# Gate and token number carried in each x row, expert outputs stored in expert order, final rows scattered

## The chip, the cores and the metric

The kernel runs on one core of a Trainium2 chip. The metric is device time of one execution, in microseconds (us), as the median of three runs. All arithmetic is float32 or float32r; each large product is made as three float32r matmuls of high and low parts.

## The reference

```python
# attention over 32 packed tokens, two softmax stages, 8 batches x 8 heads x 576 tokens x 64
p_packed = sm_attn(p, k, v)
out = sm_attn(q, p_packed, p_packed)
x = out.transpose(0, 2, 1, 3).reshape(4608, 512)
# one expert of eight for each token
logits = x @ w_gate                                   # 4608 x 8
expert_idx = argmax(logits); gate_w = softmax(logits)[expert_idx]
for e in range(8):                                    # 512 -> 1024 -> 512
    out[mask_e] = gate_w[mask_e] * (maximum(x[mask_e] @ w1[e], 0) @ w2[e])
# dense block, 512 -> 2048 -> 512
r = maximum(x @ w_in, 0); y = (s * r * r + b) @ w_out
```

## The kernel before

The program is written engine by engine, with semaphores by hand. It has three stages one behind another.

**Attention** (0 to about 185 us). Sixteen units of four heads, software-pipelined in iterations over PE (TensorE), ACT (ScalarE), DVE (VectorE) and POOL (GpSimd). A batch is two units. After each batch POOL sums its logits, DVE's `experts(b)` (L1011) picks the expert of each token by a chain of small instructions, PE ranks the tokens (`ranks`), DVE's `positions(b)` (L1030) turns ranks into row numbers, and POOL's `scatter` (L410) writes the x rows, 96 at a time and 2048 bytes each, to `x_by_expert` in DRAM: eight regions of 4736 rows. 48 such scatters run in all.

**Expert slots** (about 205 to 716 us). A slot is 128 rows of one expert; here there are 40. Behind the last tokens DVE works out tables (first slot of each expert, DRAM row of each slot), and the rows behind the last token of each region are filled with zeros: four DMAs from SP's queue (L345) and four from ACT's (L867), at addresses loaded from the table. ACT waits for all scatters and all zero rows before it loads slot 0 (`load`, L873 to L876). In the loop PE runs `slot_up(s)`, `slot_in(s + 1)`, `slot_down(s - 1)`, `slot_turn(s)`; ACT runs `relu(s)`, `x_hi(s + 1)`, `load(s + 2)`, `y_out_(s - 1)`, `h_hi(s)`; DVE makes the low parts (`x_lo`, `h_lo`). `y_out_` copies y out of PSUM and stores it at the slot's own row of `y_by_slot`. Eight chunks of the next expert's weights are split into high and low parts by POOL (`split`, L390) when an expert's buffer is released. In parallel, gate values and slot rows of all tokens are computed once and go through DRAM (`gate_dram`, `pos_dram`) so that they can be read back in token order.

**Dense** (about 725 us to the end). Nine groups of four tiles of 128 tokens. POOL gathers the y rows of a tile by token (`gather_y`, L452), ACT multiplies them by the gate (`scale`, L947), PE transposes them (`tile_in`, L723), ACT and DVE make high and low parts, then PE runs 16 blocks per group of `dense_up` and `dense_down`, 12 matmuls each. Block n needs a relu on ACT, a square on DVE (L1217), a high part on ACT (L962) and a low part on DVE (L1219). Gathers of later groups lie inside the group before. The output of a group is in token order: each partition holds four consecutive tokens, and SP writes it with one DMA of 1 MB (L367). The last weights, `w_out`, can be split only when the last slot's product is done (`release(E + 1)`).

The handover to the dense stage on ACT ends with these lines, and POOL waits for `y_all` before its first gather:

```python
y_out_(before3 + 2)
act.wait_ge(y_out, (before3 + 4) * 16)
act.sem_inc(y_all, 1)
```

## Time and profile before

| | |
|---|---|
| median of 3 runs | 1571.49 us (1571.23 to 1572.86) |
| profiled execution | 1566.7 us, of which the span of instructions is 1564.9 us |
| PE busy | 1471.0 us, 94% of the span |
| DVE, ACT, POOL busy | 471.2, 473.2, 411.2 us |
| DMA | 124.57 MB, mean 80 GB/s |
| the chain that ended last | PE 91% of it |

How to read it: PE is the engine that sets the time, so what counts is where PE is idle or runs at its lower clock. A window row gives the busy time of each engine in a stretch with its number of instructions, the granted clock as a share of 2.4 GHz, the busy share of the 16 DMA engines and the GB/s that they moved.

### The profile page before, as it was taken

The page shows a single profiled execution, that of the slowest core. Times are in us where ns is not written, and L with a number is a line of the kernel's source. Part 1 is how long each engine was busy: PE and PEld are TensorE (multiplying, and loading weights), DVE is VectorE, ACT ScalarE, POOL GpSimd, SP SyncE. Part 2 cuts the span into 40 slices and gives each one's busy share as a digit, 9 for nine tenths or more (in the row PEclk, how much of TensorE's full clock was granted, in tenths as well). Part 3 has the DMA queues.
Part 4 walks back from the last instruction along what each step waited for, and adds up shares of the span by engine and source line. Part 5 has one row for each costly group of instructions (what it writes and reads, how often), then busy time and mean ns, then how long its engine had stood idle before and what let it go on. Part 6 is the DMA issues. An engine that isn't in the chain of part 4 may idle for free.

```text
span 1564.9 us, 24350 instructions
## 1 busy us (share of the span) xinstructions
PE 1471.0 (94%) x8664; PEld 1177.8 (75%) x8665; DVE 471.2 (30%) x776; ACT 473.2 (30%) x809; POOL 411.2 (26%) x269
## 2 busy tenths in 40 slices
PE   7888369999999999995999999999999999999998
PEld 5556258888888888884788888888888888888886
DVE  3766631111111111111523232332323233232322
ACT  5655122222222222222222232322223232222222
POOL 0344568448266547006500000000000000000000
PEclk9998679999999999997999999999999999999999
DMA  8887464234233333113101010010101001000000
GB/s 260 252 263 226 136 207 161 85 107 135 75 132 107 112 123 121 67 35 108 55 8 40 14 40 7 13 40 8 39 13 40 7 13 40 8 32 0 27 1 27
DMA packets 51906, 124.57 MB, mean 80 GB/s; under 512 B 8224, under 2 KB 14368, under 8 KB 50720
## 3 DMA queue, kind: packets, MB, share of 16 engines
q1 hardware_dynamic: 31904, 83.13, 16.4%
q10 hardware_dynamic: 14016, 22.10, 4.3%
q0 software_dynamic: 5952, 18.88, 3.8%
q8 instruction: 22, 0.36, 0.1%
q14 instruction: 12, 0.10, 0.0%
HBM read 90.76 MB, written 33.33 MB: 79 GB/s over the span
## 4 chain that ended last, share of the span: by engine, by line
PE 91%; issue 3%; ACT 2%; DVE 1%; DMA 1%; POOL 0%; SPq 0%; another core or an unknown queue 0%; ACTq 0%; DVEq 0%; POOLq 0%
PE psum L660 18%; PE psum L662 18%; PE psum L661 18%; PE psum L740 9%; PE psum L742 9%; PE psum L741 9%; PE psum L493 2%; PE psum L704 2%; PE psum L728 1%; PE psum L669 1%; PE psum L554 1%; PE psum L533 1%; PE psum L608 1%; PE psum L563 0%; ACT a1T L805 0%
## 5 line engine op out<-in xcount | busy, mean ns | idle before, releaser
L1217 DVE SCALAR_TENSOR_TENSOR s_r_r<-r_relu,s_col 128x512 f32<-128x512 f32 x144 | 112.9, 784 | 453.2 <-ACT r_relu L959 453.2
L660 PE MATMUL psum<-weights_split,gT_hi 128*128 128x512 f32 x576 | 230.6, 400 | 1.9 <-DVE gT_lo L1219 1.9
L740 PE MATMUL psum<-yT_hi,weights_split 128*128 128x512 f32 x576 | 228.4, 396 | 1.4 <-issue 1.4
L741 PE MATMUL psum<-yT_lo,weights_split 128*128 128x512 f32 x576 | 228.5, 397 | 0.0
L742 PE MATMUL psum<-yT_hi,weights_split 128*128 128x512 f32 x576 | 228.4, 396 | 0.0
L662 PE MATMUL psum<-weights_split,gT_lo 128*128 128x512 f32 x576 | 228.0, 396 | 0.0
L661 PE MATMUL psum<-weights_split,gT_hi 128*128 128x512 f32 x576 | 227.6, 395 | 0.0
L959 ACT ACTIVATE r_relu<-psum 128x512 f32<-128x512 f32 x144 | 86.0, 597 | 465.5 <-PE psum L742 465.5
L395 POOL TENSOR_TENSOR weights_split<-weights_raw,one 128x1024 fp32r<-128x1024 f32 x70 | 134.7, 1925 | 252.8 <-PE psum L662 236.5
L457 POOL DMA_INDIRECT y_gathered<-y_by_slot,tpos x36 | 34.4, 957 | 580.1 <-PE psum L728 578.2
L397 POOL TENSOR_TENSOR weights_split<-weights_raw,weights_split 128x1024 fp32r<-128x1024 f32 x70 | 169.2, 2417 | 5.5
L1219 DVE SCALAR_TENSOR_TENSOR gT_lo<-s_r_r,b_col,gT_hi 128x512 fp32r<-128x512 f32 x144 | 112.9, 784 | 114.1 <-ACT gT_hi L962 114.1
L962 ACT ACTIVATE gT_hi<-s_r_r,b_col 128x512 fp32r<-128x512 f32 x144 | 104.3, 724 | 123.4 <-DVE s_r_r L1217 123.4
L660 PE MATMUL psum<-weights_split,xT_hi 128*128 x320 | 130.7, 408 | 2.9 <-DVE xT_lo L1188 2.9
L660 PE MATMUL psum<-weights_split,hT_hi 128*128 x320 | 129.8, 406 | 2.5 <-DVE hT_lo L1194 2.5
L740 PEld LDWEIGHTS psum<-yT_hi,weights_split 128*128 128x128 f32 x576 | 108.5, 188 | 28.0 <-issue 1.8
L660 PEld LDWEIGHTS psum<-weights_split,gT_hi 128*128 128x128 f32 x576 | 108.2, 188 | 27.5 <-issue 2.1
L741 PEld LDWEIGHTS psum<-yT_lo,weights_split 128*128 128x128 f32 x576 | 108.5, 188 | 26.9
L742 PEld LDWEIGHTS psum<-yT_hi,weights_split 128*128 128x128 f32 x576 | 108.7, 189 | 26.3
L662 PEld LDWEIGHTS psum<-weights_split,gT_lo 128*128 128x128 f32 x576 | 108.1, 188 | 26.1
L661 PE MATMUL psum<-weights_split,xT_hi 128*128 x320 | 127.1, 397 | 0.0
L662 PE MATMUL psum<-weights_split,xT_lo 128*128 x320 | 126.9, 397 | 0.0
(143 smaller groups left out, 1786.3 us busy)
## 6 DMA issues: line engine op xcount, KB each, us to landing
weights_raw<-in_moe_w_dram SPq DMA_DIRECT2D x64, 512.0 KB, 3.5
x_slot<-x_by_expert ACTq DMA_DIRECT2D x40, 256.0 KB, 2.7
y_by_slot<-y_slot ACTq DMA_DIRECT2D x40, 256.0 KB, 2.0
k_sb<-in_k_dram SPq DMA_DIRECT2D x16, 576.0 KB
q_sb<-in_q_dram SPq DMA_DIRECT2D x16, 576.0 KB, 7.2
v_sb<-in_v_dram SPq DMA_DIRECT2D x48, 192.0 KB
out_dram<-out_sb SPq DMA_DIRECT2D x9, 1024.0 KB, 3.9
weights_raw<-in_moe_w_in_dram SPq DMA_DIRECT2D x8, 512.0 KB, 3.7
```

Of the source, the lines that this page charges most:

```text
L395: nc.gpsimd.tensor_tensor(hi, raw[c_ % 2][:], one[:].to_broadcast([P, CH]), ALU.mult).then_inc(hi_done, 1)
L397: nc.gpsimd.tensor_tensor(lo, raw[c_ % 2][:], hi, ALU.subtract).then_inc(conv, 1)
L660: nc.tensor.matmul(dst, lhs[0][:, col:col + P], rhs[0], start=first_, stop=False)
L661: nc.tensor.matmul(dst, lhs[0][:, col:col + P], rhs[1], start=False, stop=False)
L662: return nc.tensor.matmul(dst, lhs[1][:, col:col + P], rhs[0], start=False, stop=last_)
L740: nc.tensor.matmul(ps[:, HFB + f % 2, :], w[0], yT[0][:, k_, :], start=(k_ == 0), stop=False)
L741: nc.tensor.matmul(ps[:, HFB + f % 2, :], w[0], yT[1][:, k_, :], start=False, stop=False)
L742: last = nc.tensor.matmul(ps[:, HFB + f % 2, :], w[1], yT[0][:, k_, :], start=False, stop=(k_ == KD - 1))
L959: nc.scalar.activation(rel[:], ps[:, HFB + par, :], ACT.Relu).then_inc(rel_done, 1)
L962: nc.scalar.activation(gT[par][0][:], sq[par][:], ACT.Identity, bias=b_col[:]).then_inc(ghi_done, 1)
L1217: nc.vector.scalar_tensor_tensor(sq[par][:], rel[:], s_col[:], rel[:], ALU.mult, ALU.mult).then_inc(sq_done, 1)
L1219: nc.vector.scalar_tensor_tensor(gT[par][1][:], sq[par][:], b_col[:], gT[par][0][:], ALU.add, ALU.subtract).then_inc(glo_done, 1)
```

## The change

The last two columns of a longer x row (514 floats, 2056 bytes) hold the gate and the token's output row number. The gate is computed batch by batch in the attention stage. A y row (513 floats, 2052 bytes) is scaled when it leaves PSUM and carries the row number. The y rows are stored without gaps in expert order: a slot that would reach beyond its expert's last token starts earlier, so that no padding rows are read (as long as an expert has 128 tokens or more). The dense stage reads contiguous tiles with plain DMAs, and its result rows are scattered to the output by POOL. Zero rows are written once, at the head of each region, before the attention loop. The first four tiles are loaded, transposed and split while the last slots are still in work.

```diff
-    rows_dram = nc.dram_tensor("x_by_expert", [E * REG, DM], F32).ap()
-    ys_dram = nc.dram_tensor("y_by_slot", [SLOTS * P, DM], F32).ap()
-    pos_dram, gate_dram = ...
+    rows_dram = nc.dram_tensor("x_by_expert", [E * REG, XW], F32).ap()   # XW = DM + 2
+    ys_dram = nc.dram_tensor("y_sorted", [N + P, YW], F32).ap()          # YW = DM + 1
@@ SP, after the attention loads
-            sp.wait_ge(rt, RT_PAD)
-            for e in range(E // 2):
-                row = sp.value_load(pad_row[0:1, e:e + 1], ...)
-                sp.dma_start(rows_dram[bass.ds(row, P), :], zeros[:]).then_inc(zeroed, 16)
-            sp.dma_start(ys_dram[N:SLOTS * P, :]..., zeros[:]...).then_inc(tail_zero, 16)
@@ SP, dense
+            for c_ in range(2):
+                chunk(c_, (E + 1) * NCH + c_, w_out_chunk(c_))
+            sp.wait_ge(y_out, before3 * 16 + 16)
+            for i in range(GT):
+                load_y(1, i)
+            for c_ in range(2, NCH):
+                chunk(c_, (E + 1) * NCH + c_, w_out_chunk(c_))
+            for g in range(2, GROUPS):
+                for i in range(GT):
+                    load_y(g, i)        # waits for ty_full of the tile before
-            with sp.Fori(0, GROUPS) as g:
-                sp.dma_start(out_v[:, bass.ds(g, 1), :], osb[:]...).then_inc(out_done, 16)
@@ POOL scatter
+                if j0 == 0:
+                    nc.gpsimd.tensor_copy(x_rows[:, b % XBUFS, :, DM + 1], ids[:, b, :]).then_inc(ids_done, 1)
@@ POOL, end
-            (gather_y(0), split 1, gather_y(1), splits 2 to 7, gather_y(2 to 8))
+            for c_ in range(NCH):
+                split(c_, (E + 1) * NCH + c_, WBUF)
+            for g in range(GROUPS):
+                for i in range(GT):
+                    pool.wait_ge(o_dve if i % 2 else o_act, 2 * g + 3 + i // 2)
+                    nc.gpsimd.indirect_dma_start(out, IndirectOffsetOnAxis(ap=out_row[:, t:t + 1], axis=0), osb[:, i, :], None)
+                pool.wait_ge(out_done, 16 * GT * (g + 1))
+                pool.sem_inc(osb_free, 1)
@@ PE, end of the slots
             slot_up(before3 + 2)
+            tile_in(0, 0)
+            tile_in(0, 1)
             slot_down(before3 + 1)
+            tile_in(0, 2)
+            tile_in(0, 3)
             slot_turn(before3 + 2)
             slot_down(before3 + 2)
-            for i in range(GT):
-                tile_in(0, i)
@@ ACT
+            act.dma_start(rows_dram.rearrange("(e r) c -> r e c", e=E)[0:P],
+                          zeros[:].unsqueeze(1).to_broadcast([P, E, XW])).then_inc(zeroed, 16)
+                if it >= 5 and it % 2 == 1:
+                    exp_logits((it - 5) // 2)
-            def y_out_(s):
+            def y_out_(s, age):
+                nc.scalar.copy(ysb[:, DM:], gid[age][:, 1:2])
-                nc.scalar.copy(ysb[:], ps[:, YB, :]).then_inc(y_done, 1)
+                nc.scalar.activation(ysb[:, 0:DM], ps[:, YB, :], ACT.Copy, scale=gid[age][:, 0:1]).then_inc(y_done, 1)
                 act.wait_ge(y_done, s + 2)
+                row = act.value_load(y_at[0:1, bass.ds(s, 1)], min_val=0, max_val=N)
+            def keep_columns(s, n):     # n copies of 128x2 between three buffers, then one out of x_slot
@@ DVE
@@ experts(b)
+                nc.vector.tensor_tensor(shifted[:], lgb, mx[:]..., ALU.subtract).then_inc(exp_in, 1)
+            def gates(b):               # at the head of positions(b)
+                nc.vector.reduce_sum(psum_e[:], powers[:], AX.X)
+                nc.vector.tensor_scalar_add(psum_e[:], psum_e[:], EPS)
+                nc.vector.reciprocal(x_rows[:, b % XBUFS, :, DM], psum_e[:])
```

Three places in the order of instructions (a wait on a semaphore stands in brackets; x3 is three in a row).

ACT between attention and slots, before. The names: `x_slot` is the tile of slot 0, `el` and `dl` belong to the gates of all tokens.

```order
L867 DMA x_by_expert<-zeros 128x512
L901 TENSOR_LOAD slots_minus [waits tables]
L875 TENSOR_LOAD slot_row [waits x_sent3,x_sent2,zeroed,x_sent1,x_sent0]
L876 DMA x_slot<-x_by_expert 128x512
L829 CAST weights_split<-weights_raw 128x1024 [waits raw_in0]
L829 CAST weights_split<-weights_raw 128x1024 [waits raw_in1]
L910 ACTIVATE el<-dl 96x384 [waits rt]
L880 CAST xT_hi<-psum 128x512 [waits tx_full]
```

The same place of the changed kernel.

```order
L832 ACTIVATE logits_exp<-logits_shifted 96x48 [waits exp_in] x2
L912 TENSOR_LOAD slots_minus [waits tables]
L876 TENSOR_LOAD slot_row [waits x_sent2,x_sent3,x_sent1,x_sent0]
L877 DMA x_slot<-x_by_expert 128x514
L828 CAST weights_split<-weights_raw 128x1024 [waits raw_in0]
L828 CAST weights_split<-weights_raw 128x1024 [waits raw_in1]
L881 CAST xT_hi<-psum 128x512 [waits tx_full]
L908 COPY gate_and_token<-x_slot 128x2
```

The zero DMAs and the wait on `zeroed` are gone from here; two small exponentials stand in their place.

PE from the last slot's `slot_up` to the dense stage, before: `xT` rows are `slot_up`, `hT` rows `slot_down`, `h_relu` rows `slot_turn`.

```order
L704 MATMUL psum<-ident,h_relu 128x128 [waits hlo_done,relu_done]
L704 MATMUL psum<-ident,h_relu 128x128 x3
L660 ISA [waits y_done,hlo_done,conv]
L660 MATMUL psum<-weights_split,hT_hi 128x512
...
L728 MATMUL psum<-ident,y_gathered 128x128 [waits yg_scaled]
L728 MATMUL psum<-ident,y_gathered 128x128 x3
L728 MATMUL psum<-ident,y_gathered 128x128 [waits ylo_done,yg_scaled]
L740 MATMUL psum<-yT_hi,weights_split 128x512 [waits rel_done,ylo_done,conv]
```

The same of the changed kernel.

```order
L719 MATMUL psum<-ident,y_tile 128x128 [waits row_read]
L719 MATMUL psum<-ident,y_tile 128x128 x3
...
L657 ISA [waits y_done,hlo_done]
L657 MATMUL psum<-weights_split,hT_hi 128x512
...
L719 MATMUL psum<-ident,y_tile 128x128 [waits ylo_done,row_read]
...
L701 MATMUL psum<-ident,h_relu 128x128 [waits hlo_done,relu_done]
...
L657 ISA [waits y_done,hlo_done,conv]
...
L731 MATMUL psum<-yT_hi,weights_split 128x512 [waits rel_done,ylo_done,conv]
```

The sixteen transposes of group 0 moved ahead of the last slot's `slot_down`, eight before and eight after that of the slot before it.

ACT over the same stretch in the changed kernel, from the load of the four tiles on; before, the copies to `y_slot` were followed directly by the DMA and by `hT_hi`.

```order
L939 DMA y_tile<-y_sorted 128x513 x4
L891 CAST hT_hi<-psum 128x512 [waits th_full] x2
L886 ACTIVATE h_relu<-psum 128x512 [waits h_full]
L946 CAST out_row_of_y<-y_tile 128x1 [waits yg_in0]
...
L950 CAST yT_hi<-psum 128x4x128 [waits ty_full] x2
L897 COPY y_slot<-gate_and_token 128x1 [waits y_out]
L898 ACTIVATE y_slot<-psum,gate_and_token 128x512
L900 TENSOR_LOAD slot_y_row
L901 DMA y_sorted<-y_slot 128x513
L950 CAST yT_hi<-psum 128x4x128 [waits ty_full] x2
L891 CAST hT_hi<-psum 128x512 [waits th_full] x2
```

Ahead of the last `hT_hi` there now stand the load of a row number and two more `yT_hi`.

## Rows read from the trace of the kernel before

**Rows 1.** Busy time by stretch, core 0.
```profile
160.00:200.00 40.00, 11.47 (x240) 9.11 (x237) 21.83 (x71) 3.90 (x7) 21.57 (x25) 0.58 0.50 156
200.00:240.00 40.00, 29.77 (x133) 23.98 (x134) 14.83 (x17) 10.75 (x18) 30.21 (x15) 0.82 0.58 185
500.00:600.00 100.00, 100.00 (x482) 81.95 (x481) 15.84 (x24) 26.70 (x48) 56.04 (x27) 1.00 0.34 110
700.00:720.00 20.00, 13.26 (x61) 10.30 (x59) 1.29 (x2) 2.84 (x5) 4.07 (x2) 0.98 0.07 27
```

**Rows 2.** The chain that ended last, slots to dense: start, length, what.
```profile
707.80 0.59 ACT hT_hi L890
...
709.92 0.49 PE psum L660
...
715.53 0.25 PE psum L662
...
744.59 0.48 PE psum L660
```

**Rows 3.** Timeline around the second last slots: start, length, engine, line.
```profile
694.59 0.59 ACT L896 COPY y_slot<-psum 128x512 f32<-128x512 f32 x1 [5.04 <-PE psum L662]
696.35 1.29 DVE L1194 TENSOR_TENSOR hT_lo<-psum,hT_hi 128x512 fp32r<-128x512 f32 x2 [6.08 <-ACT hT_hi L890]
700.97 0.60 ACT L885 ACTIVATE h_relu<-psum 128x512 f32<-128x512 f32 x1 [2.20 <-PE psum L662]
706.37 1.03 PE L704 MATMUL psum<-ident,h_relu 128*128 128x128 f32 x8
743.75 2.34 POOL L395 TENSOR_TENSOR weights_split<-weights_raw,one 128x1024 fp32r<-128x1024 f32 x1
744.27 2.38 DVE L1217 SCALAR_TENSOR_TENSOR s_r_r<-r_relu,s_col 128x512 f32<-128x512 f32 x1
```

**Rows 4.** Small operations by line, or a line's own answer: count, durations.
```profile
L821 ACT COPY pkx<-psum 128x8 f32<-128x8 f32 x16 | 2.5, 158 | 0.5 <-PE psum L544 0.5
L950 ACT ACTIVATE y_gathered<-y_gathered,tgate 128x512 f32<-128x512 f32 x36 | 25.6, 711 | 7.9 <-DMA y_gathered<-y_by_slot,tpos 7.9
L875 ACTq TENSOR_LOAD <-slot_row x40: 274/277/994, 199.9 to 676.5; - x40
```

**Rows 5.** Attention to slots: the last scatter (timeline), then the chain.
```profile
192.93 0.92 POOL L414 DMA_INDIRECT x_by_expert<-x_rows,row_of_token_sb  x1 [0.30 <-issue]
...
195.84 4.01 DMA x_by_expert<-zeros
...
201.33 5.97 DMA x_slot<-x_by_expert
...
210.06 0.79 PE psum L660
```

**Rows 6.** DMAs issue to landing: of x_slot, of y_gathered, and two issues by line.
```profile
DMA to landing us min/median/max: 2.4/2.7/6.0
DMA to landing us min/median/max: 3.1/3.3/4.0
y_by_slot<-y_slot ACTq DMA_DIRECT2D x40, 256.0 KB, 2.0
out_dram<-out_sb SPq DMA_DIRECT2D x9, 1024.0 KB, 3.9
```

**Rows 7.** Attention: chain of one odd iteration, and two stretches of its start.
```profile
91.56 0.22 DVE eq L1019
...
25.00:30.00 5.00, 4.02 (x82) 3.22 (x80) 2.18 (x5) 2.90 (x5) 0.00 (x0) 0.87 0.26 91
10.00:15.00 5.00, 3.44 (x40) 2.53 (x38) 1.18 (x2) 2.87 (x5) 0.00 (x0) 1.00 1.07 320
```

**Rows 8.** The end: last copy of a result tile (timeline), and POOL's gathers by line.
```profile
1559.75 0.69 DVE L1226 COPY out_sb<-psum 128x512 f32<-128x512 f32 x1 [0.64 <-PE psum L662]
...
L457 POOL DMA_INDIRECT y_gathered<-y_by_slot,tpos x36 | 34.4, 957 | 580.1 <-PE psum L728 578.2 <-issue 1.7
```

271 lines of the change are left out of this document (132 added, 139 removed).

## The prediction

> **What bounds the kernel now.** I read the windows by stage first. In the middle of the slots PE is busy 100.00 of 100 us at granted clock 1.00, so nothing is won there by work taken off other engines. PE is idle in two places: between attention and slots (11.47 us busy of 40, then 29.77 of 40) and between slots and dense (13.26 busy of 20 in the first half of that gap) [rows 1]. The dense stage behind it is as full as the slots: the product chain there is PE's alone. Then I read the chain that ended last across both gaps, and the timelines for what each engine does in them.
>
> In the second gap the turn of the last slot begins at 706.37 [rows 3]; PE starts the last y product at 709.92, ends it at 715.78, and starts the first dense down product at 744.59 [rows 2]. In between stand the store of y, a weight split on POOL, the gather, and four rounds of scale, transpose and copy one behind another, none overlapped. In the first gap the last scatter starts at 192.93, the last zero DMA at 195.84 and lands 4.01 us later, slot 0's load starts at 201.33, takes 5.97 us, and PE's first slot product starts at 210.06 [rows 5].
>
> All sums are made against the profiled execution: 1566.7 us, its span 1564.9 us. The median of the three runs is 1571.49, 4.8 us more; I add my difference to that median.
>
> **Slots to dense, the main term.** New timetable, on the old trace's clock. PE ends `slot_up` of the last slot as before; its second relu runs 700.97 to 701.57 [rows 3]. The first tile's transposes wait for that relu and a cast of 128x1, priced as the 128x8 copy at 0.158 [rows 4], so they start at 701.8, 1.1 after PE was free. Eight transposes cost 1.03 like the eight of the turn [rows 3]. That puts `slot_down` of the slot before last 2.1 later: its end moves from 706.4 to 708.5. Two more tiles (1.03) and the turn (1.03) follow, then PE waits for `h_lo`. On ACT: 0.1 to see the product, 0.16 for the row-number column, 0.71 for the scaled copy (the scale of a y tile has the same shape, 0.711 [rows 4]), 0.17 for its semaphore, a row load of 0.28 [rows 4] with about 0.4 of register work, 0.35 for the DMA, two `yT_hi` of 0.59 like the y copy [rows 3]: `hT_hi` starts 3.35 after the product. Before, it took 2.12 from there to PE's start (707.80 to 709.92 [rows 2]); I add 0.2 because DVE has `y_lo` to finish. Last y product: starts 714.2, takes 5.86, ends 720.1. The two dense up blocks take 5.6 (24 matmuls, like the y product without its start) and end at 725.7.
>
> The first down block cannot start then: its relu, square, high and low part need 3.0 us after the first up block, and POOL is splitting `w_out` from 720.2 on. In the trace a DVE instruction with both inputs in SBUF that started at 744.27, during a POOL split that ran from 743.75 to 746.09, ended at 746.65, 2.38 instead of 0.75 [rows 3]: it waited for the POOL instruction to end. With splits of 1.9 and 2.35 in turn the square and the low part each lose about a microsecond: down starts at 727.3. Against 744.59 that is **17.3 us gained**. Bounds: 19.8 with no POOL wait and one microsecond less on ACT; 12.7 with both waits at 2.38, half a microsecond more on ACT, and PE's clock down after the idle stretch.
>
> That last point is open. PE is now idle for some 3.6 us in one piece, where before a 2.5 us piece at 707.4 left the clock at 0.98 over its stretch [rows 1] and the long gap lowered it. A fall would cost 12 matmuls 0.2 us each, 2.4 in all. I leave it out of the sum and keep it in the range.
>
> **Attention to slots.** Zero rows and the wait on them are gone from here. The last scatter starts 0.4 later (POOL copies ids, one small instruction and its semaphore), 193.3. Its landing is not shown. The gather of the same queue and nearly the same size lands in 3.3 (3.1 to 4.0), a plain store of y in 2.0 [rows 6]; I take the gather's 3.3, since the queue is the same. With 0.7 for the row load, slot 0's load starts at 197.4. Its 5.97 was in company of zero stores and weights; the median is 2.7 [rows 6], and now the stores are gone and weight chunk 9 came earlier: 200.1. From landing to PE's first product 2.7 as before: 202.8 against 210.06, **7.2 us gained**. Bounds: 8.5 with landing in 2.0; 3.2 if scatter and load take 4.0 and 6.0.
>
> The table step on DVE grows by five or so instructions of 0.2 on one partition; it ended before the last scatter was issued and has until that lands, so it costs nothing. Without that cover it would cost 1 us.
>
> **Attention loop.** `experts(b)` stands on the chain, one small DVE instruction after another at 0.22 to 0.24 [rows 7]. One more is added, for seven batches inside the loop: **1.7 us lost**. The three of `gates(b)` (0.6 together) go between an x copy and the turn of the packs, behind which DVE waited for PE in the iteration that I followed (90 to 105 us), so they are hidden; unhidden they would cost 0.6 x 7 = 4.2. The exponential on ACT falls into a wait for PE.
>
> The zero rows are written at 12 us: 1024 rows of 2056 bytes, 2.1 MB. DMA moves 320 GB/s with a share of 1.07 there, but at 25 to 30 us the share is 0.26 [rows 7], and k, q, v are loaded an iteration ahead. I take **0.5 us lost**, including ACT's time to issue it; 0 if it is all hidden, 2.1 MB / 0.29 = 7.2 if not at all.
>
> **Slot loop.** Zero. ACT gets per slot three copies of 0.16, the column, 0.12 more in the scaled copy and a row load: about 1.8 us. The one path that matters is y product, y copy, `h_hi`, `h_lo`: its low parts ended at 697.64, and PE wants them at about 701.3, after `slot_up` and `slot_in` [rows 3]. The path grows by 0.95 and had 3.7 to spare.
>
> **Dense loop and end.** Gathers leave POOL, tile loads leave from SP, ACT saves 0.55 per tile, POOL scatters. None is on PE's chain, and osb is free 80 us before it is wanted. Zero. If the scatter of a group were held up, PE would wait only from 80 us on. At the very end SP's 1 MB store landed 3.9 after its issue [rows 6], 0.2 after the last copy ended at 1560.44 [rows 8]. Now POOL issues four scatters, 0.957 each [rows 8] with 0.3 between; tiles come every 0.8, so the fourth starts at about 1562.15 and lands 2.6 to 3.3 later, 1564.75 to 1565.45 against 1564.55. I take **0.6 lost**, -0.4 to 1.6.
>
> **Sum.** -17.3 - 7.2 + 1.7 + 0.5 + 0.6 = -21.7 us. The span goes to 1543.2, the profiled execution to 1545.0, the median to 1549.8.
>
> **Two rules weighed.** Above, the zero store was hidden by the gap in DMA traffic at 25 us. The Trainium skill (DMA: Bandwidth & Descriptors, Issuing engines are not separate DMA queues) says that DMAs from any engine share the same 16 DMA engines and interleave, so ACT's queue buys nothing but issue time. By that rule alone the sum would be -21.7 + 6.7 = -15.0. Whether loads are late for it no row before can show; that is rival A.
>
> The x rows grow by 0.4% in bytes. The same page (How a descriptor splits into AXI transactions) says that a descriptor that does not start on a 256-byte boundary is cut into more transactions; nearly every 2056-byte row starts off one. By it the estimate is some 10% more DMA work for the scatters, 0.06 MB per batch or 0.2 us, 1.8 us if attention were bound by DMA. No run so far shows it.
>
> **Rivals.**
> A. *Attention is held by DMA.* DMA engines stood at a share of 1.07 just when the zero store would be issued [rows 7]. If loads come late, the zero store costs up to 7.2 and longer rows 1 or 2 more. For it: the share. Against it: in the waits of the loop PE is released by ACT and DVE, hardly ever by a load. Time: 1549.8 + 4 to 8 = 1554 to 1558. Chance 0.2.
> B. *The handover is worse than my timetable*: clock falls (2.4), POOL blocks DVE for two or three blocks more (1.5 each), scatter lands late (2). For it: the 2.38 row. Time 1553 to 1557. Chance 0.13.
> C. *Slower.* ACT's longer round in the slot loop reaches PE. It decides once the path y product to `h_lo` grows by more than 3.7 us per slot; then each microsecond beyond costs 37. A row load once took 0.99 instead of 0.277 [rows 4], which would bring the growth to 1.7, still 2 short. One microsecond beyond gives 1549.8 + 37 = 1587. Chance 0.03.
> D. *The gap is moved, not closed.* The tiles' loads or the new waits (SP's on y stores, PE's on `row_read`) hold PE before the last slot's products, and the first gap is set by scatters that land no sooner: gains of 3 and 3 instead of 24. About 1568. Chance 0.04.
> The forecast itself: 0.6, with its own range 1546.5 to 1553.5.
>
> **Numbers.** Predicted 1549.8. 80% range: from 1545.5 (bounds 19.8 and 8.5, no losses but 1.7) to 1558 (rivals A and B inside). 0.2%, about 3.1 us, is what a measurement of this kernel can tell. Faster 0.94, same 0.02, slower 0.04.
>
> **What the changed kernel's profile would show.** Slots to dense: from the end of the second last y product to the first down product about 18.8 us instead of 38; a PE idle piece of 3 to 4 us before the last y product, its releaser `hT_lo`; clock 1.00 through it. Attention to slots: `x_slot` load about 3.5 to 4 us after the last scatter, landing in 2.7. Attention: iterations with `experts` 0.2 longer, the last scatter about 2.5 later than 192.93. Slots: windows still 100.00 of 100. End: last scatter issued at about 1.7 after the last copy. I am wrong if the attention stage is more than 5 us longer, if PE has idle time between slots 5 and 35, or if the first down product waits more than 3 us for `gT_lo`.

## The result and the profile after

The changed kernel takes 1560.22 us (median of 4 runs, 1558.07 to 1561.81) against 1571.41 for the kernel before on the same chip: ratio 0.9928, interval 0.9915 to 0.994. It is 11.2 us faster, where 21.7 was forecast, and lies above the range. The profiled execution took 1560.72 us, its span 1559.0, against 1566.7 and 1564.9: 5.9 us less by the pair of profiles. The profile of before had caught a quick execution, 4.8 us under its median. One of ten later executions of the kernel before (run before_again) took 2110.83 us at a granted clock of 0.648 and is left out of that run's ratio.

I cut both traces at five marks: the start of the last scatter, the start of the first slot product, the start of the last relu of the slots, the start of the first dense down product, the end of the last result copy. In us:

| stretch | before | after | difference | forecast | difference of means |
|---|---|---|---|---|---|
| attention, to the last scatter | 192.93 | 204.13 | +11.2 | +2.6 | +9.5 |
| to the first slot product | 17.13 | 9.61 | -7.5 | -7.6 | -8.2 |
| slots, to the last relu | 490.91 | 492.69 | +1.8 | 0 | +0.9 |
| to the first dense down product | 43.62 | 29.12 | -14.5 | -17.3 | -15.5 |
| dense, to the last result copy | 815.85 | 811.51 | -4.3 | 0 | -4.6 |
| end | 4.46 | 11.94 | +7.5 | +0.6 | +7.5 |
| sum | | | -5.8 | -21.7 | -10.4 |

The last column takes four profiles of before or of near variants of it (before, before_again, before_zero, before_aligned) and five of the changed kernel (after, after_again, end_nowait, end_plain, handover; handover only up to the last relu, and of the end only after and after_again). Two of the four have an edit in a stage of the table: without before_zero the attention difference is +9.1; without before_aligned the one to the first dense down product is -14.9 and the dense one -5.0. The means add up to -10.4, next to the measured -11.2. Two profiles of one kernel differ by 1 to 3 us in the attention stage alone, so a single pair would have left 5 us unexplained here.

Busy time by stretch in the changed kernel (as in rows 1):

```profile
160.00:200.00 40.00, 20.48 (x405) 15.95 (x403) 29.18 (x99) 9.74 (x20) 21.21 (x26) 0.63 0.31 95
200.00:240.00 40.00, 26.12 (x112) 20.88 (x113) 9.18 (x19) 9.70 (x21) 29.15 (x16) 0.76 0.48 149
500.00:600.00 100.00, 100.00 (x481) 81.63 (x480) 15.85 (x24) 31.86 (x81) 55.71 (x28) 1.00 0.36 115
700.00:720.00 20.00, 15.09 (x80) 12.07 (x77) 4.83 (x8) 7.37 (x18) 0.00 (x0) 1.00 0.43 132
720.00:740.00 20.00, 17.37 (x67) 13.78 (x68) 7.21 (x5) 3.39 (x7) 11.68 (x6) 0.91 0.18 60
```

In the slots PE is still busy 100.00 of 100, with ACT at 31.86 us instead of 26.70 [rows 1]: ACT's longer round doesn't reach PE. The second gap, between slots and dense, has shrunk to one idle piece. The clock stays at 1.00 up to 720 and is 0.91 in the stretch behind.

The chain across the first gap, from the attention stage to the slots (start, length, what; as in rows 5):

```profile
204.13 3.40 DMA x_by_expert<-x_rows,row_of_token_sb
...
208.34 2.65 DMA x_slot<-x_by_expert
...
213.74 0.79 PE psum L657
```

Landing 3.40 for the scatter (3.3 taken from the gather), 2.65 for the load (2.7 taken): this term was read rightly.

The chain across the second gap (as in rows 2), then the last copy and the last scatter in the timeline (as in rows 8):

```profile
715.07 0.87 PE psum L719 x8
715.94 0.87 PE psum L701 x8
716.81 3.78 issue
720.59 0.49 PE psum L657
...
722.15 0.43 PE psum L658
...
731.43 1.58 DVE s_r_r L1224
...
733.80 1.52 DVE gT_lo L1226
...
735.55 0.47 PE psum L657
```

```profile
1546.37 0.69 DVE L1233 COPY out_sb<-psum 128x512 f32<-128x512 f32 x1 [0.64 <-PE psum L659]
...
1548.98 0.96 POOL L465 DMA_INDIRECT out_dram<-out_sb,out_row_of_y  x1 [0.30 <-issue]
```

The last copy ends at 1547.06. The last scatter starts 1.92 later, about as forecast (1.7). But the span ends only at 1559.0. The windows of the changed kernel (columns as in rows 1) say that nothing is left to do for most of that:

```profile
1550.00:1552.00 2.00, 0.00 (x0) 0.00 (x0) 0.00 (x0) 0.00 (x0) 0.00 (x0) 0.66 0.35 131
1552.00:1558.00 6.00, 0.00 (x0) 0.00 (x0) 0.00 (x0) 0.00 (x0) 0.00 (x0) 0.50 0.00 0
```

No engine works and no DMA moves from 1552 on. Two things thus had to be explained above all: the 7.5 us at the end, and 6.9 us more than forecast in attention.

### The profile page after: what moved, and what is told of

Its sections match the earlier page's. It is cut to its first block, busy times and chain, and to the rows that moved or that the text cites. A ratio compares the mean times of both kernels' runs of the same rounds, so it can differ in the third digit from the quotient of the medians.

```text
span 1559.0 us, 24694 instructions
## 1 busy us (share of the span) xinstructions
PE 1468.7 (94%) x8664; PEld 1181.3 (76%) x8665; DVE 474.2 (30%) x808; ACT 480.7 (31%) x973; POOL 416.0 (27%) x278
## 4 chain that ended last, share of the span: by engine, by line
PE 90%; DVE 3%; issue 2%; DMA 1%; ACT 1%; POOL 1%; another core or an unknown queue 0%; SPq 0%; ACTq 0%; DVEq 0%; POOLq 0%
PE psum L657 18%; PE psum L659 18%; PE psum L658 18%; PE psum L733 8%; PE psum L732 8%; PE psum L731 8%; PE psum L701 2%; PE psum L490 2%; PE psum L666 1%; PE psum L719 1%; PE psum L551 1%; PE psum L530 1%; PE psum L592 1%; DMA q_sb<-in_q_dram 1%; PE psum L605 1%
## 5 line engine op out<-in xcount | busy, mean ns | idle before, releaser
L1224 DVE SCALAR_TENSOR_TENSOR s_r_r<-r_relu,s_col 128x512 f32<-128x512 f32 x144 | 116.2, 807 | 449.5 <-ACT r_relu L955 449.5
L465 POOL DMA_INDIRECT out_dram<-out_sb,out_row_of_y x36 | 35.6, 990 | 746.9 <-ACT out_sb L965 738.6
L657 PE MATMUL psum<-weights_split,hT_hi 128*128 x320 | 130.8, 409 | 4.7 <-issue 4.7
L1206 DVE TENSOR_TENSOR hT_lo<-psum,hT_hi 128x512 fp32r<-128x512 f32 x80 | 51.6, 686 | 265.4 <-ACT hT_hi L891 265.4
L658 PE MATMUL psum<-weights_split,hT_hi 128*128 x320 | 127.1, 397 | 0.0
```

The costliest lines, as they stand in the source:

```text
L657: nc.tensor.matmul(dst, lhs[0][:, col:col + P], rhs[0], start=first_, stop=False)
L658: nc.tensor.matmul(dst, lhs[0][:, col:col + P], rhs[1], start=False, stop=False)
L1224: nc.vector.scalar_tensor_tensor(sq[par][:], rel[:], s_col[:], rel[:], ALU.mult, ALU.mult).then_inc(sq_done, 1)
```

## Experiments

Each run has its median and its ratio to runs of the kernel before on the same chip, with the 95% interval of the ratio. In one of the five series (pad160, before_moved, gates_late, two_edits) the attention stage ran nearly throughout at the upper clock, and all kernels were some 20 us shorter, the kernel before at a median of 1549.35; those four are compared with each other and by their ratios.

### How far one profile may be trusted

**before_again** is the kernel before, unchanged, profiled once more.

> The kernel before, once more, as a yardstick. Its profiled execution took 1566.7 us and its timed runs 1571.2 to 1572.9. If the profiled one was simply a fast one, the runs here spread between 1566 and 1573 and their granted clock with them (0.966 for the profiled one); if the profile differs by a fixed mechanism, all timed runs stay at 1571 to 1573 and the clock or one stage shows why. In the profile I expect the last scatter at 193 and the last result copy to end 4.5 us before the span does.

1571.53 us, ratio 0.9991 (0.9977 to 1.0006); the last scatter starts at 195.93 instead of 192.93, the handover to the dense stage takes 45.65 instead of 43.62. **after_again** is the changed kernel, unchanged.

> The changed kernel once more, on the same chip as the run below, since two profiles of one kernel differ by up to 3 us in the attention stage, and a whole series can lie 20 us from another with the clock. Theory: ratio to the kernel before 0.9928 as before, within 0.0015; 11.9 us at the end, 29.1 at the handover, 811.5 to 812 in the dense stage, whatever the clock does in the attention stage. If the attention stage runs at its upper clock nearly throughout, as it did in the last series, the gate costs the loop more, some 1.1 us a batch, and the ratio is 0.994 to 0.995.

1558.32 us, 0.9913 (0.9898 to 0.9929); last scatter at 203.44, end 11.95. The ratio of the change stands; the stages move by a few microseconds between executions, the end doesn't.

### The end

**end_nowait** takes away POOL's wait for its last four scatters; SP waits for them anyway.

```diff
-                pool.wait_ge(out_done, 16 * GT * (g + 1))
-                pool.sem_inc(osb_free, 1)
+                if g < GROUPS - 1:
+                    pool.wait_ge(out_done, 16 * GT * (g + 1))
+                    pool.sem_inc(osb_free, 1)
```

> The changed kernel with POOL's last wait for its own scatters left out (SP alone waits for them before the end; nobody needs osb any more). In the trace of the changed kernel the last scattered bytes moved at 1551.9, but the span ends at 1559.0, and SP waited 7.0 us for another engine's end. Theory 1 (POOL has something to do at its end that takes about 7 us, and it can start only when its wait is over): the end now starts 3 us earlier and the time is 1557. Rival 1 (what takes 7 us begins when the last scatter has landed, whoever waits): 1560, no change. Rival 2 (the 7 us are the wait of POOL itself for its semaphore): the span ends 1 us after the last bytes, 1553.5.

**end_plain** stores the last group by one plain DMA of SP instead, without a scatter; POOL's last scatter lies 80 us earlier.

```diff
+            sp.wait_ge(o_act, 2 * GROUPS + 2)
+            sp.wait_ge(o_dve, 2 * GROUPS + 2)
+            sp.dma_start(out[(GROUPS - 1) * GT * P:GROUPS * GT * P, :]..., osb[:]).then_inc(sb_in, 16)
...
-            for g in range(GROUPS):
+            for g in range(GROUPS - 1):
```

> The changed kernel with the last group written by one plain DMA of 1 MB from SP instead of POOL's four scatters (its 512 rows land in the wrong places of the output). POOL's last scatter is then that of the group before, 80 us from the end. Theory (POOL is late because its program ends only some 7 us after its last scatter has run): from the end of the last copy to the end of the span it takes 4.5 us as in the kernel before, instead of 11.9, and the time is 1560.2 - 7.5 = 1552.7. Rival (the 7 us come from something else in the new ending, such as SP's wait on 36 scatters): 11 us and 1559.

end_nowait: 1557.63 us, 0.9911 (0.9888 to 0.9934), from last copy to span end 10.07. end_plain: 1552.89 us, 0.9875 (0.9825 to 0.9924), 4.87 from last copy to end, about as in the kernel before (4.46). SP's queue waits (releaser, total us, count, longest), first of the changed kernel:

```profile
SPq L62 <- PEq L62: 7.0, 1, 7.0
```

then of end_nowait:

```profile
SPq L62 <- PEq L62: 5.2, 1, 5.2
```

then of end_plain:

```profile
SPq L372 <- DMA out_dram<-out_sb: 3.9, 1, 3.9
...
SPq L62 <- PEq L62: 0.2, 1, 0.2
```

L62 is the end of the program, where the engines wait for each other. In the kernel before this wait is 0.2 as well. The row names PE's queue, but PE's last matmul had started at 1545.94. What the wait is for shows in the instructions of line 62 on POOL's queue (duration in ns, start in us), of the changed kernel:

```profile
L62 POOLq DRAIN  x1: 6932/6932/6932, 1551.8 to 1551.8; - x1
```

of end_nowait:

```profile
L62 POOLq DRAIN  x1: 9769/9769/9769, 1545.1 to 1545.1; - x1
```

of end_plain:

```profile
L62 POOLq DRAIN  x1: 6606/6606/6606, 1466.4 to 1466.4; - x1
```

and of the kernel before, with POOL's last gather (timeline):

```profile
L62 POOLq DRAIN  x1: 8112/8112/8112, 1367.2 to 1367.2; - x1
...
1367.41 0.94 POOL L457 DMA_INDIRECT y_gathered<-y_by_slot,tpos  x1 [21.88 <-PE psum L728]
```

In end_nowait POOL's last scatter begins here (timeline):

```profile
1546.95 0.96 POOL L465 DMA_INDIRECT out_dram<-out_sb,out_row_of_y  x1 [0.30 <-issue]
```

In line 62 this DRAIN stands ahead of the last two semaphore instructions of POOL's queue. In the changed kernel it starts when the wait for the landing is over, at 1551.8, lasts 6.9 us, and the span ends 0.2 later. In end_nowait it is in the queue early and ends 6.9 us after the last scatter (1547.91 to 1554.9), again 0.2 before the span's end; the last scatter had landed by 1549.7, so the 6.9 us don't run from the landing. Dropping the wait let them start 2 us earlier and saved 1.9. In the kernel before the same DRAIN ends 6.9 us after the last gather (1368.36 to 1375.3), 190 us before the end, and in end_plain 79 us before it; there nobody waits for it. So POOL needs some 6.9 us behind its last gather or scatter before the program can end. What it does in them the trace doesn't show, and since POOL's last work is a gather or a scatter in every kernel here, no run shows whether other work would leave the same.

### Attention: the gates

**no_gates** leaves out the shift, the exponential and the three instructions of `gates`.

```diff
+                        nc.gpsimd.memset(x_rows[:, b % XBUFS, :, DM], 1.0)     # b < XBUFS
-                    exp_logits((it - 5) // 2)
-                nc.vector.tensor_tensor(shifted[:], lgb, mx[:]..., ALU.subtract).then_inc(exp_in, 1)
-                gates(b)
```

> The changed kernel without the gate's arithmetic in the attention stage: no shifted logits, no exponential, no sum, epsilon and reciprocal (the gate column is a constant 1 set four times by POOL, so the expert outputs are not scaled). Theory 1 (all four DVE instructions of a batch stand on the loop's chain, 0.8 us a batch, and 1.4 in the drain): last scatter at 204.1 - 6.5 = 197.6, time 1553.5. Rival, my prediction's term (only the one in experts is on the chain): 1.7 less, last scatter at 202.4, time 1558.5. Rival 2 (the loop is held by loads that come late): nothing changes, 204.

1555.24 us, 0.9887 (0.9864 to 0.991), where the changed kernel has 0.9928 and 0.9913: 4 to 6.5 us less by the ratios. The last scatter starts at 200.83. I split the stage by loads of v: to that of unit 7, from there to unit 15 (four batches), and to the last scatter.

| | before (mean of 4) | changed (mean of 5) | no_gates | three_edits |
|---|---|---|---|---|
| to v of unit 7 | 64.5 | 68.3 | 70.3 | 68.6 |
| units 7 to 15 | 81.7 | 84.1 | 81.6 | 81.1 |
| to the last scatter | 47.6 | 50.8 | 49.0 | 49.2 |

The first row scatters between 66.9 and 69.6 in the five profiles of the changed kernel, and the middle row between 80.1 and 84.2 in the four of before, so a single profile says little here; no_gates and three_edits (described below, with two of the gate's instructions fewer) agree in the middle row. Read by these means, the gates are the whole of the middle row's 2.4 and more than half of the last row's 3.2: some 4.4 us, against 1.7 forecast, with a few us of uncertainty.

The changed kernel's own chain (start, length, what) holds the three instructions of `gates` four times, here first:

```profile
124.99 0.12 DVE sum_of_exp L1044
...
125.13 0.18 DVE sum_of_exp L1046
...
125.33 0.19 DVE x_rows L1049
```

The others begin at 145.59, 167.28 and 184.79, and the shift of the logits is on the chain five times at 0.20: 3 us in all. In the iteration around 104 us the three are not on it, and DVE waits 1.14 us for PE behind them, as in the one that the prediction had followed. So they are hidden in some batches and not in others.

**gates_late** moves `gates` behind the turn of the packs, where DVE had waited for PE in the iteration that I had followed. **two_edits** is the changed kernel with end_nowait's and handover's edits, its gates unchanged.

```diff
@@ gates_late
-                gates(b)                      # at the head of positions(b)
...
+                if it >= 5 and it % 2 == 1 and it < UNITS + 2:
+                    gates((it - 5) // 2)      # behind turn_packs(it - 2)
```

> The changed kernel with the sum, the epsilon and the reciprocal of the gate moved behind DVE's transpose of the packs, where DVE waits 1.1 us for PE, instead of ahead of it; the last batch's stay ahead of its positions. POOL's scatters wait for them. Without the gate's arithmetic the loop took 20.4 us a batch instead of 21.0, and 49.0 instead of 50.9 from the last v load to the last scatter. Theory 1 (the three cost because they delay the transpose and what waits for it): a batch 20.6, last scatter 201.5, time 1558. Rival (they cost wherever they stand, or the shifted logits in experts are what costs): a batch 21.0, last scatter 203.3, time 1560.

> The changed kernel with the two edits that helped alone and leave the tiles where they are: the last h ahead of tiles 2 and 3 at the handover, and no last wait on POOL. 29.1 becomes 28.2 and 11.9 becomes 10.1: time 1557.4, ratio to the kernel before 0.991, and 0.989 if the better medians of the two runs alone (0.9895 and 0.9911) mean more than their profiles.

gates_late 1540.04 us, 0.9943 (0.9924 to 0.9963), last scatter at 185.34; two_edits 1535.05 us, 0.9923 (0.9894 to 0.9952), 180.22. Behind the turn the gates do no better. two_edits has two savings at other places that gates_late lacks, some 3 us or 0.0019, and the four middle batches take 68.7 us in it against 70.9 in gates_late. The chain of two_edits shows what the gates hold up:

```profile
94.52 0.76 DVE nm L1066
95.28 0.86 DVE x_rows L1113
96.14 0.12 DVE sum_of_exp L1045
...
96.28 0.18 DVE sum_of_exp L1047
...
96.48 0.19 DVE x_rows L1050
...
97.10 0.79 DVE a2T L1091
...
99.13 1.25 PE psum L593 x48
```

The three instructions stand between an x copy and `a2T`, which PE's 48 matmuls wait for. In this iteration, at the upper clock, DVE has no wait to spare.

**gates_pool** has POOL make shift, sum and reciprocal, for all batches but the last, with tiles of 224 bytes more:

```diff
+                nc.gpsimd.tensor_tensor(half[:], powers[:, :, 0:4], powers[:, :, 4:8], ALU.add).then_inc(pool_sum, 1)
+                ...                                       # quarter, whole, + EPS, pow(-1)
-                gates(b)
+                if b == B - 1:
+                    gates(b)
```

> The changed kernel with the gate's arithmetic of the first seven batches on POOL (one subtraction, three additions, epsilon, a power of -1; the exponential stays on ACT; the last batch stays on DVE), and the row numbers written into the x rows one step ahead, out of the way of the scatters. Theory 1 (what the four DVE instructions and POOL's copy cost is their place on DVE's and POOL's chain; without the arithmetic at all the last scatter came at 200.8 instead of 203.3 on average): last scatter at 200 to 201, time 1557. Rival (POOL's five instructions hold DVE's, as its splits do, or delay the scatters): last scatter at 203 or later, time 1560 or more.

1565.28 us, 0.9958 (0.9944 to 0.9973): last scatter at 204.94, no sooner than with the work on DVE. **best** is gates_pool with the edits of end_nowait and handover.

> The three edits together on the changed kernel: the gates on POOL, the last h ahead of tiles 2 and 3 at the handover, and no last wait on POOL. The handover edit alone gave 28.2 us from the last relu to the first down product instead of 29.1, the edit of the end 10.1 us from the last copy to the end of the span instead of 11.9. If they add up to what the gates give: 1560.2 - 3 - 1 - 1.9 = 1554.3, ratio to the kernel before 0.989. Rival (the gates on POOL give nothing): 1557.3, ratio 0.991.

1560.24 us, 0.9937 (0.9922 to 0.9953), last scatter at 204.58. My expectation that POOL had room fell. Why POOL's scatters are no sooner was not taken apart. Both kernels also lost 4.5 to 5.6 us in the dense stage (817.15 and 816.02), of which below.

### Attention: the zero rows and the longer rows

**zero_spread** writes the zeros by eight DMAs from SP's queue between the loads of units 2 to 5; **zero_spread2** does the same and lets POOL wait for them only before its first scatter.

```diff
+                if u <= 5:
+                    for e in (2 * u - 4, 2 * u - 3):
+                        sp.dma_start(rows_dram[e * REG:e * REG + P, :], zeros[:]).then_inc(zeroed, 16)
-            act.dma_start(rows_dram.rearrange("(e r) c -> r e c", e=E)[0:P], ...)
```

> The changed kernel with the same zero rows written by eight DMAs of 0.26 MB from SP, two behind the loads of each of the units 2 to 5, instead of one DMA of 2.1 MB from ACT at 12 us. Theory 1 (the single big store delayed the q load of unit 2, which took 11.8 us, and with it the loop by about 3 us): PE no longer waits for q at 33 us, the last scatter starts at 201 instead of 204.1 and the time is 1557, 3 less. Rival (the bytes themselves cost, wherever they are written, since the DMA engines are the limit of the loop): last scatter at 203.5 to 204.5, time 1560.

> As the kernel that spread the zero rows over eight DMAs behind the loads of units 2 to 5, but POOL waits for them only before its first scatter and no longer before it sums the logits of batch 0. In the first version that wait held POOL until 55.9 us (18.3 us idle) and the fifth load mark came 3 us later than in the changed kernel. Theory 1 (the big store delayed the loads and with them the loop by about 3 us; spread out it costs 1): v load of unit 6 issued at 54 to 55 us instead of 57.5, last scatter at 201, time 1557.5. Rival (the bytes cost the same wherever they are written): last scatter at 203 to 204, time 1560.

1564.66 us, 0.9958 (0.9941 to 0.9975), last scatter at 207.42; and 1563.34 us, 0.994 (0.9923 to 0.9958), 205.91. Neither is faster than the single store (0.9928 and 0.9913); zero_spread is slower, while zero_spread2's interval touches the changed kernel's. POOL's wait (timeline of zero_spread) is one reason, gone in the second:

```profile
55.89 0.59 POOL L409 TENSOR_TENSOR lg<-head_logits 96x192 f32<-96x192 f32 x1 [18.26 <-DMA x_by_expert<-zeros]
```

The chain of zero_spread has a slow q load too, 11.27 us at 29.61, as if the delay had only moved with the stores; that is a reading and not a test.

**before_zero** adds the single early store, in rows of 2048 bytes, to the kernel before, and POOL waits for it ahead of its loop; nothing else changes.

```diff
+            act.wait_ge(zeros_done, 1)
+            act.dma_start(rows_dram.rearrange("(e r) c -> r e c", e=E)[0:P], zeros[:]...).then_inc(early_zero, 16)
```

> The kernel before with one thing of the change added: the same single DMA of zero rows (1024 rows, here of 2048 bytes) from ACT at 12 us, and POOL waiting for it before the loop; its own late zero rows stay as they are. In four profiles of kernels with the early store the v load of unit 6 went out at 54.9 to 57.9 us, in two without it at 52.3 and 53.1; the last scatter at 202.2 to 204.1 against 192.9 and 195.9, but there the gate's arithmetic is in it too. Theory 1 (the store costs the loop about 3 us, once, and what is left of the difference is the gate's): unit 6 at 55 to 57, last scatter at 197.5, time 1575, 3 above the kernel before. Rival 1 (it is hidden, my prediction's 0.5): 194.5 and 1572. Rival 2 (2.1 MB at the full rate): 201, 1579.

1572.65 us, 1.0015 (1.0 to 1.0029): between nothing and 4.5 us, best value 2.4. In its trace v of unit 7 is loaded at 65.74 instead of 64.33, but the last scatter starts at 192.84, where it was. In the changed kernel the store is issued at 12.02 and lands 17.3 us later. A q load that goes out while it is under way takes 11.78 us (in before_zero 10.25; the median of the 16 q loads in the kernel before is 7.2), and the chain runs through it:

```profile
21.55 11.78 DMA q_sb<-in_q_dram
33.33 0.14 issue
33.47 1.51 PE psum L490 x6
```

**rows512** keeps the longer row in SBUF but scatters and loads 2048 bytes of it.

```diff
-                                                 x_rows[:, b % XBUFS, j], None).then_inc(x_sent[b % XBUFS], 16)
+                                                 x_rows[:, b % XBUFS, j, 0:DM], None).then_inc(x_sent[b % XBUFS], 16)
```

> The changed kernel with x rows of 512 floats in DRAM, scattered and loaded without the two columns (gate 1 and the row number of the slot position are put into the tile once, and the output rows are a plain count, so the outputs are neither scaled nor in place; both columns are still computed). Theory 1 (2056-byte rows that start off the 256-byte boundaries cost the DMA engines more, and the attention loop feels it): last scatter 2 us earlier than 204, time 1558. Rival (row length and start don't matter to the loop): last scatter 203 to 204.5, and the load of a slot still takes 2.7 us; time 1560.

1564.45 us, 0.9941 (0.9923 to 0.9959), last scatter at 204.28, slot 0's load lands in 2.7 in both. The longer x rows cost nothing that shows. (Its dense stage is 4.8 us longer, as in the kernels with moved tiles, of which below.) The y rows of 2052 bytes are another matter, and no run gives them back their old length. Their store lands in 3.0 us, where that of 2048 bytes took 2.0 [rows 6]:

```profile
y_sorted<-y_slot ACTq DMA_DIRECT2D x40, 256.5 KB, 3.0
```

Whether the length of the row does it is not shown.

### Slots to dense

**handover** moves the last turn ahead of the last two tiles on PE, and `h_hi` and `h_lo` ahead of their copies on ACT and DVE.

```diff
             slot_down(before3 + 1)
+            slot_turn(before3 + 2)
             tile_in(0, 2)
             tile_in(0, 3)
-            slot_turn(before3 + 2)
...                                   # and the same on ACT and DVE
```

> The changed kernel with the last turn of h ahead of the transposes of tiles 2 and 3 on PE, and the high and low parts of h ahead of those two tiles' on ACT and DVE. In the changed kernel PE sits idle 3.8 us before the last y product and then runs 12 matmuls at half clock. Theory (the idle piece has two instructions of ACT and two of DVE too many, and the clock fell because it was that long): idle 2.4, the y product 5.9 to 6.1 instead of 7.25, last relu to first down product 26.3 instead of 29.1, time 1557.4. Rival (the clock falls after 2.4 us of idle time as well): 27.7 and 1558.8. Second rival (the y_lo of tiles 2 and 3 come late now and hold the dense stage's first up block): 29, no change.

1557.68 us, 0.9895 (0.9854 to 0.9936); the stretch is 28.24 instead of 29.12. Its chain:

```profile
715.35 2.46 issue
717.81 0.49 PE psum L657
...
719.96 0.43 PE psum L658
```

The idle piece shrinks by 1.3 us, but matmuls of 0.43 instead of 0.23 still come behind it, and the last y product takes 7.43 us, as in the changed kernel (7.41): with a pause of 2.46 the clock fell as well. The first rival came.

### Dense: where the 4.3 us came from

In the changed kernel the twelve up matmuls of a block, four to a line, differ by line (from 760 to 1500 us; count, busy us, mean ns):

```profile
L733 PE MATMUL psum<-yT_hi,weights_split 128*128 128x512 f32 x522 | 206.0, 395 | 0.0
L731 PE MATMUL psum<-yT_hi,weights_split 128*128 128x512 f32 x523 | 204.9, 392 | 0.0
L732 PE MATMUL psum<-yT_lo,weights_split 128*128 128x512 f32 x522 | 204.3, 391 | 0.0
```

In before all three take 395. Each line has 576 matmuls in the stage, so 3 and 4 ns less on two of them are some 4 us, which is the difference to explain. **pad160** puts 160 bytes of unused tile ahead of the dense stage's tiles.

```diff
+        sb("pad", [P, 40])
         out_row = sb("out_row_of_y", [P, TOK], I32)
```

> The changed kernel with nothing but 160 bytes per partition left empty in SBUF ahead of the tiles of the slot and dense stages, so that each of them starts 160 bytes later. Theory (where the dense stage's tiles start in SBUF sets the rate of its up blocks; in the changed kernel they start 448 bytes beyond a multiple of 512, in the two kernels of mine that were moved by 160 and 224 bytes the three matmuls of an up block all took 395 to 396 ns): 395 to 396 for all three instead of 392, 391 and 395, first down product to last copy 816 instead of 811.5, time 1564.7. Rival (something else in those two kernels did it, such as the missing gate or the work put on POOL): 811.5 and 1560.2.

1544.08 us, 0.9973 (0.9958 to 0.9989). Its dense stage takes 816.35 and its three lines read:

```profile
L732 PE MATMUL psum<-yT_hi,weights_split 128*128 128x512 f32 x520 | 205.9, 396 | 0.0
...
L733 PE MATMUL psum<-yT_lo,weights_split 128*128 128x512 f32 x519 | 205.4, 396 | 0.0
L734 PE MATMUL psum<-yT_hi,weights_split 128*128 128x512 f32 x519 | 205.4, 396 | 0.0
```

In the eleven profiles of the changed kernel and its variants whose tiles lie where its own do, the stage takes 811.1 to 813.6 us; in the four with tiles moved (pad160, rows512, gates_pool, best) 816.0 to 817.2. So it isn't the new way of loading tiles that made the stage shorter, but where the tiles came to lie in SBUF. I tried to give this to the kernel before. **before_aligned** pads by 32 bytes so that `yT` starts at a multiple of 64; **before_moved** pads by 800, so that it starts at the changed kernel's remainder by 2048.

> The kernel before with a pad of 32 bytes per partition ahead of the tables in SBUF, so that yT, gT, xT and hT start on multiples of 64 bytes instead of 32 beyond one; nothing else. In the changed kernel they are on multiples of 64 and two of the three matmuls of an up block of the dense stage took 391 and 392 ns, in the kernel before all three 395; in the run with short x rows, which has 144 bytes more ahead of them, they took 396 again and the dense stage 816.3 us instead of 811.5. Theory (the start of the moving operand in SBUF sets it): 391 to 392 for two of the three matmuls, first down product to last copy 811.5 to 813.5 instead of 815.9 to 818.0, the time 4 lower, 1568. Rival (it comes from something else in the changed kernel's dense stage, such as its loads or its place in the code): 395 for all, time unchanged at 1572.

> The kernel before with 800 bytes per partition left empty in SBUF ahead of the tables, so that yT, gT, xT and hT start as far beyond a multiple of 2048 (1984) as they do in the changed kernel. 32 bytes, which put them on multiples of 64, left all three matmuls of an up block at 394 to 395 ns. Theory (the start of the tile alone sets it): 391 to 392 for two of three, dense stage 811.5 to 813, time 1567. Rival (it takes more than the start of these tiles, for instance how the tiles that ACT and DVE write lie to those that PE reads, which differ between the kernels): 395 and 815 to 816, time 1571.

1568.38 us, 0.9979 (0.9965 to 0.9994), dense 814.81; and 1548.45 us, 0.9996 (0.9977 to 1.0015), dense 815.00. Both have 395, 395 and 394 ns, and their dense stage is at best 1 us of the 4.3 shorter. The start of `yT` alone, by either rule, isn't what decides. The cause stays open beyond "placement".

### All together

**three_edits** has end_nowait's and handover's edits, and the row carries the sum of the exponentials instead of the gate. `+ EPS` and the reciprocal are done once per slot on DVE, 128 rows at a time, in the slot loop where DVE has room.

```diff
-                nc.vector.reduce_sum(psum_e[:], powers[:], AX.X).then_inc(gate_of, 1)
-                nc.vector.tensor_scalar_add(psum_e[:], psum_e[:], EPS).then_inc(gate_of, 1)
-                nc.vector.reciprocal(x_rows[:, b % XBUFS, :, DM], psum_e[:])
+                nc.vector.reduce_sum(x_rows[:, b % XBUFS, :, DM], powers[:], AX.X)
+            def turn_sum(s):     # at the head of x_lo(s)
+                nc.vector.tensor_scalar_add(xin[:, DM:DM + 1], xin[:, DM:DM + 1], EPS).then_inc(gate_of, 1)
+                nc.vector.reciprocal(xin[:, DM:DM + 1], xin[:, DM:DM + 1]).then_inc(gate_of, 1)
```

> The kernel of the two edits with a third: the x row carries the sum of the exponentials instead of the gate, and DVE adds epsilon and takes the reciprocal once per slot (two instructions on 128x1, before the low part of x), so that a batch of the attention stage has two instructions fewer on DVE. No tile moves. Theory (every DVE instruction of the gate counts in full where the loop is bound by DVE's chain; in the profile of the two edits all three stood on it, 0.53 us of sum, epsilon and reciprocal): 0.4 us less a batch, 3 to 3.5 us less at the last scatter, ratio to the kernel before 0.990 where the two edits gave 0.9923, and 0.003 below the changed kernel's on the same chip at the least. Rival (the loop takes back what DVE saves, since PE at half clock is its bound for most of the stage): ratio as with two edits, 0.992. Second rival (ACT's copies of the columns now wait for DVE and come late in the slot loop): slots more than 493 us from the first product to the last relu.

1551.13 us (1550.3 to 1552.07), 0.9865 (0.9849 to 0.9882). By its ratio it is the fastest kernel of the study, 7.2 us below the changed kernel in the same series, and it does all of the reference's work. Last scatter at 198.82, slots 491.68 (491.1 to 492.7 in the other variants of the changed kernel), handover 27.79, end 10.10, dense still 811.16. By the marks, against the changed kernel's means, the end is 1.8 us shorter, the handover 1.8 and the attention stage 4.5.

## Why the prediction was wrong

The mechanism was right where the change was meant to work: the two gaps gave 23.7 us of the 24.9 forecast. Two stages priced at 2.6 and 0.6 us lost 9.5 and 7.5, and 4.6 came back by luck. By the differences of means, against the forecast's terms:

- **Dense loop and end, "I take 0.6 lost": this step failed first, by 6.9 us.** The scatters' issue and landing were right (the last one starts 1.92 after the last copy and has landed at 1551.7, 2.7 later). The sum took the landing for the end of the program. In its place comes POOL's DRAIN of 6.9 us behind its last work: end_plain removes the cost, end_nowait shows that it runs from POOL's last scatter and not from the data. The trace of the kernel before had this DRAIN, 8.11 us long and ended 6.9 after the last gather, but 190 us from the end, where it cost nothing; the rows that the term was drawn from don't hold it.
- **Attention loop, "they are hidden": this step failed, by 2.7 us.** The gates cost about 4.4 and not 1.7. I had followed one iteration (90 to 105 us) and found DVE waiting for PE. The changed kernel has such an iteration too, at 104 us, but in four of the eight batches the chain runs through all three instructions. My own price for "unhidden" was 4.2 + 1.7 = 5.9; the truth lay nearer to it. gates_late shows that the other place tried doesn't hide them either, and three_edits that fewer instructions do help: the last scatter comes 4.5 earlier than the changed kernel's mean.
- **The rest of attention.** Of the 9.5 us the gates are 4.4, and at most some 1.4 of the last row are left beside them. The id copy on POOL lies there, ahead of the last scatters: the last nine take 10.8 us instead of 9.9, one of them 1.75 instead of 0.92. The first row's 3.9 has the zero store in it: before_zero shows 1.7 at that mark and none at the last scatter, 2.4 (0 to 4.5) by its times. "0.5 lost" was low but within that interval. Some 2 us at the start stay open: PE pauses for 2.96 us at 54.3 in the changed kernel, 1.59 before, and before_zero and before_aligned have 2.7 and 2.4 there as well.
- **Slots to dense, -17.3: right in kind, 2.8 too large** by the pair, 1.8 by the means. From the end of the second last y product to the first down product it is 20.5 us, forecast 18.8. 1.55 of it is the clock: eight matmuls of 0.41 to 0.43 behind the idle 3.78 (forecast 3.6), so that the y product takes 7.41 instead of 5.86. I had named it, priced it at 2.4 and left it out of the sum. It belonged in: the gap before [rows 1] had already shown 0.82 and 0.98 behind idle stretches. 0.96 more is a wait of PE ahead of `slot_down` of the slot before last, at 708.25, which my timetable didn't have. DVE's two stretched instructions, 1.58 and 1.52 instead of 0.75 each, came as forecast from the 2.38 row.
- **Attention to slots, -7.6 with its 0.4 of ids: right.** 7.5 by the pair, 8.2 by the means.
- **Slot loop, 0: nearly right**, +0.9 by the means and 1.8 by the pair. Rival C didn't happen.
- **Dense loop, 0: wrong in sign**, 4.6 gained, by a placement that nobody chose. Without this accident the change would have won some 6.6 us and not 11.2; pad160, which is the change without it, has 0.9973 (0.9958 to 0.9989), 4.2 us, at the upper clock. This was luck, and it hid part of the error.

Of the rivals, A (DMA holds attention) had the right stage and the wrong cause: before_zero and rows512 leave it 2 us or so of its 4 to 8. On the rule of the Trainium skill (DMA: Bandwidth & Descriptors, Issuing engines are not separate DMA queues): the q load of 11.78 us beside the store, 10.25 in before_zero, agrees that they share the DMA engines; that sharing didn't hold the stage up by the 7.2 us which it would have at worst, 1.7 at the mark of unit 7 in before_zero. On the same page of the Trainium skill (How a descriptor splits into AXI transactions): rows512 against the changed kernel shows no cost of 2056-byte rows where my estimate was 1.8 us if DMA were the bound. By [rows 6] against the changed kernel the store of y, in rows of 2052 bytes, is 1.0 us longer, which would fit the rule, but no run tests it. (The estimate of 1.8 us has a slip: a batch's x rows are 1.18 MB, 10% of them 0.12 MB and not 0.06, so it should have been some 3.3 us.) B (a worse handover) came in part: the clock fell, the scatter was not late. D fell: both gaps closed as far as they were meant to. The sign of what would make me wrong, attention more than 5 us longer, is the one that came.

The range missed because each term's bound was drawn from rows of its own operation, and the end had no bound for what POOL does behind its last scatter. Two smaller slips change nothing: by its own terms (-19.8 - 8.5 + 1.7) the range starts at 1544.9 and not 1545.5, and the 0.29 MB per us of the zero store stands in no row shown; with the 320 GB/s of [rows 7] its 7.2 us are 6.6.

## What to carry to other kernels

- If a change moves an engine's last work to the end of the program, the end has to be priced for itself: look in the old trace at what that engine's queue does behind its last instruction, also where nobody waits for it. Here one plain store of SP ended the program 7 us sooner than POOL's scatters; but in end_plain its rows land in the wrong places, so it shows the price and is no remedy for an output that must be scattered. Dropping POOL's needless last wait is one, worth 1.9.
- A few small instructions are hidden only if the engine waits in every iteration at that place; one iteration read in the trace doesn't say so. Count the engine's small instructions per batch, and where they stand on the chain, move them to a stage that has room (here the slot loop, once per slot); moving them to POOL within the attention stage brought nothing.
- When the products of a stage weren't touched and it changes by half a per cent, compare the mean of its commonest instruction before looking for a mechanism: new tiles move all that are allocated behind them.

## What was unexpected of the hardware

- POOL's queue has a DRAIN at the end of the program that ends 6.9 us after POOL's last gather or scatter (kernel before, end_nowait), or takes 6.9 us itself when POOL has first waited for the landing (changed kernel). The final wait of the other engines for it is 0.2 us when it lies 80 us or more back, and the row of that wait names PE's queue, not POOL's.
- The same float32r matmul of 128x512 takes 391 or 396 ns on average by the placement of tiles in SBUF, and 160 bytes decide (811.5 against 816.35 us of dense stage). Neither a multiple of 64 nor the same remainder by 2048 of `yT`'s start brought it.
- An idle piece of 2.46 us of PE at clock 1.00 was followed by matmuls at the lower level (0.43 instead of 0.23 us) 1.73 us after PE had started again; behind one of 3.78 they came after 0.73.
- In one series the attention stage of the kernel before (in before_moved) started its last scatter at 168.14 instead of 193, on a chip on which an earlier series had run at the lower level. two_edits has the ratio 0.9923 (0.9894 to 0.9952) there; of the changed kernel itself that series has no run. Its window from 60 to 140 us, in before_moved, which has granted clock 1.00 where before's profile had 0.91:

```profile
60.00:140.00 80.00, 71.07 (x1639) 52.12 (x1631) 69.39 (x167) 57.69 (x113) 45.72 (x48) 1.00 0.97 294
```

DVE and ACT did more work in the same 80 us too (in before's profile 56.84 and 47.41 us). Why the clock was granted there is open.
